# Order of products in a fused attention, MLP and expert kernel on one Trainium2 core: an up product moved across the group boundary, a transpose moved inside an expert tile, a weight split moved behind it

## The reference

```python
attn_out = _attn_ref(**attn_kwargs)          # 2 x 8 heads, 768 positions, head_dim 64; 8 global keys, 96 local ones
x = transpose(attn_out) -> (1536, 512)
h = x @ w_in                                 # (1536, 2048)
g = np.maximum(h, 0.0) + alpha * np.minimum(h, 0.0)
x = g @ w_out                                # (1536, 512)
logits = x @ w_gate + modality_bias[modality_id]     # 8 experts
e_idx = np.argmax(logits, axis=1)            # each token goes to one expert
gate_w = softmax(logits)[token, e_idx]
for e in range(8):
    mask = e_idx == e
    h = np.maximum(x[mask] @ w1[e], 0.0)     # 512 -> 1024
    out[mask] = gate_w[mask, None] * (h @ w2[e])     # 1024 -> 512
```

## Time and profile before

| what | value |
|---|---|
| median of 3 runs | 594.56 us (593.52 to 595.53) |
| the profiled execution's own time | 593.55 us |
| its span, first to last instruction | 591.8 us |
| PE busy | 577.8 us, 98% of the span |
| PE weight loads busy | 485.5 us, 82% |
| DVE busy | 331.5 us, 56% |
| ACT busy | 187.1 us, 32% |
| POOL busy | 122.0 us, 21% |
| mean granted TensorE clock | 0.997 |

### The profile page before, as it was taken

The page is one execution under the profiler, slowest core; times in us unless marked ns, Lnnn a source line. Parts: engine busy times, 40 slices in busy tenths (PEclk is TensorE's granted clock), DMA queues, the critical chain, the costliest instruction groups (busy, mean ns, idle before and its releaser), DMA issues.

```text
span 591.8 us, 10667 instructions
## 1 busy us (share of the span) xinstructions
PE 577.8 (98%) x3305; PEld 485.5 (82%) x3306; DVE 331.5 (56%) x852; ACT 187.1 (32%) x435; POOL 122.0 (21%) x187
## 2 busy tenths in 40 slices
PE   8999999999999999999999999999999999999995
PEld 4777778888989999899988999877778787877874
DVE  5877888787544465444554568775221289721211
ACT  4888887442010000100001004131221377521121
POOL 4444544997000000000000000101211113211110
PEclk9999999999999999999999999999999999999998
DMA  7976642562010000100001008014511169211110
GB/s 151 198 151 101 148 122 62 154 190 85 1 54 1 0 1 1 53 0 0 0 0 54 1 0 285 18 54 157 218 53 35 35 189 358 95 53 36 35 53 16
DMA packets 74544, 47.63 MB, mean 80 GB/s; under 512 B 52751, under 2 KB 60943, under 8 KB 74512
## 3 DMA queue, kind: packets, MB, share of 16 engines
q1 hardware_dynamic: 70288, 39.50, 23.9%
q0 software_dynamic: 2480, 7.34, 3.8%
q10 hardware_dynamic: 1744, 0.39, 0.3%
HBM read 40.93 MB, written 7.08 MB: 81 GB/s over the span
## 4 chain that ended last, share of the span: by engine, by line
PE 90%; DVE 5%; DMA 2%; issue 2%; ACT 1%; DVEq 0%
PE wide L1247 12%; PE wide L1249 11%; PE wide L1248 11%; PE wide L1235 9%; PE bank L1247 9%; PE bank L1249 9%; PE bank L1248 9%; PE bank L1407 4%; PE wide L1482 4%; PE bank L1507 4%; PE bank L1410 2%; DMA xg<-x_scratch,src_i 2%; PE wide L1346 2%; PE wide L1242 1%; PE bank L1495 1%
## 5 line engine op out<-in xcount | busy, mean ns | idle before, releaser
L865 DVE TENSOR_SCALAR h_act<-bank,alpha_sb 128x384 f32<-128x384 f32 x62 | 38.3, 617 | 106.3 <-PE bank L1249 106.3
L1247 PE MATMUL bank<-x_hl,wts 128*128 (+1 forms) x248 | 85.3, 344 | 0.0
L1249 PE MATMUL bank<-x_hl,wts 128*128 (+1 forms) x248 | 83.6, 337 | 0.0
L1248 PE MATMUL bank<-x_hl,wts 128*128 (+1 forms) x248 | 83.3, 336 | 0.0
L1247 PE MATMUL wide<-wts,h_h 128*128 128x512 f32 x192 | 75.7, 394 | 2.3 <-DVE h_l L868 2.3
L1249 PE MATMUL wide<-wts,h_l 128*128 128x512 f32 x192 | 75.9, 395 | 0.0
L1248 PE MATMUL wide<-wts,h_h 128*128 128x512 f32 x192 | 75.7, 394 | 0.0
L1124 DVE TENSOR_TENSOR hg_l<-wide,hg_h 128x256 fp32r<-128x256 f32 (+1 forms) x45 | 21.7, 510 | 59.8 <-ACT hg_h L605 59.5
L1247 PE MATMUL wide<-wts,hg_h 128*128 (+1 forms) x120 | 51.3, 427 | 0.2
L756 POOL DMA_INDIRECT xg<-x_scratch,source x1 | 1.9, 1920 | 226.9 <-DVE source L1021 226.9
L1247 PEld LDWEIGHTS bank<-x_hl,wts 128*128 128x128 f32 x248 | 46.6, 188 | 1.7
(11 more groups left out here) (217 smaller groups left out, 1040.0 us busy)
## 6 DMA issues: line engine op xcount, KB each, us to landing
stage<-in_moe_w SPq DMA_DIRECT2D x32, 512.0 KB, 7.5
ring<-in_moe_w_in SPq DMA_DIRECT2D x16, 256.0 KB, 2.9
ring<-in_moe_w_out SPq DMA_DIRECT2D x16, 256.0 KB, 2.9
v_raw<-in_v SPq DMA_DIRECT2D x16, 192.0 KB, 2.8
x_scratch<-x2row SPq DMA_DIRECT2D x4, 768.0 KB, 3.8
k_raw<-in_k SPq DMA_DIRECT2D x14, 192.0 KB, 3.3
q_raw<-in_q SPq DMA_DIRECT2D x14, 192.0 KB, 3.9
v_win<-in_v SPq DMA_DIRECT2D x16, 96.0 KB, 2.6
```

What stands on the lines that cost most here:

```text
L865: link(ts(h, acc, 0.0, alpha_sb[:, j:j + 1], ALU.min, ALU.mult))
L1247: pe.matmul(acc, lhs[0], rhs[0], start=start, stop=False)
L1248: pe.matmul(acc, lhs[0], rhs[1], start=False, stop=False)
L1249: return pe.matmul(acc, lhs[1], rhs[0], start=False, stop=stop)
```

## The change

```diff
@@ DVE, one expert tile
                 split(0)
                 hidden_low(t, 0)
-                split(1, 2)
+                split(1)
                 gathered_low(t + 1)
                 hidden_low(t, 1)
-                split(3, 4, 5, 6, 7)
+                split(2, 3, 4, 5, 6, 7)
                 scaled(t)
@@ PE, one MLP group
                     nxt = lambda j: up(g, j, order0[j] if first else j, banks[j % 2], first)
-                    if not first:
-                        nxt(0)
                     for j in range(FC):
                         if j + 1 < FC and not (first and j < 2 * AHEAD - 1):
                             nxt(j + 1)
+                        if j == FC - 1 and not last:
+                            up(g + 1, 0, 0, banks[0])
                         if j == 0:
                             pe.wait_ge(x2_copied, 2 * g + 2)
                         down(j)
@@ PE, one expert tile
                     pe.wait_ge(y_copied, t + 1)
                     pe.wait_ge(hg_low, 3 * t + 1)
-                    down_part(t, o, range(2))
+                    down_part(t, o, [0])
                     turn_h(t, 1)
-                    down_part(t, o, range(2, 4))
+                    down_part(t, o, range(1, 4))
                     pe.wait_ge(hg_low, 3 * t + 2)
```

## The result

| | before | after |
|---|---|---|
| median | 594.04 us (592.14 to 595.53, 4 runs) | 587.01 us (585.98 to 587.63, 4 runs) |
| profiled execution, its span | 593.55, 591.8 us | 586.40, 584.5 us |
| PE busy | 577.8 us | 570.6 us |

The ratio is 0.9886 with an interval of 0.9866 to 0.9905, that is 5.6 to 8.0 us. The direction is as forecast; the size is not: 7.0 us came off where 5.1 were forecast, and 587.01 lies 1.0 us under the low end of the range, 588.0. Of the 2.4 us between 587.01 and the 589.4 forecast, 0.5 come from the median of before, which a fourth run moved from 594.56 to 594.04.

The account below looks back on a forecast made before the run. The prediction took PE, busy 98% of the span, as the bound, so only gaps in its stream could pay. Gains of 2.8 + 2.1 + 0.2 = 5.1 us off 594.56 gave 589.4 us, range 588.0 to 592.0.

Parts of the forecast that it names:

- Part 2: Looped tiles: transposes three matmuls earlier close the stop at down chunk 4, 0.19 us in eleven ordinary tiles, 2.1 us.
- It is a wait: Down chunk 4 of looped tiles: the load, 0.30 us late, waits for DVE's low part, though the page says "issue".
- Part 1: MLP group boundaries: an up product moved across closes two stops, 0.94 us at each of three, 2.8 us.
- the copies' wait: Group boundary: ACT's accumulator copies, covered by up(1) alone, just fit; cost 0, bounds 0 and 0.3 us a boundary.
- The moved transposes: Looped tiles: ACT's hidden row reaches them in time; cost 0, bounds 0 and 0.1 us a tile.
- (b): Looped tiles: earlier transposes only move the wait and the tiles give nothing; 591.8 us, chance 0.10.
- (c): Group boundary: the wait for accumulator copies replaces both stops, and the tiles give nothing; 594.6 us, chance 0.08.
- Part 3: Three fresh tiles: split 2 later on DVE; together they give 0.2 us instead of 0.57.
- The refill: Fresh tiles: SP's later load of the next expert's piece 2 costs 0, upper bound 1.4 us.
- (a): Second fresh tile: the load of piece 2 is late by its upper bound, 1.4 us; 590.8 us, chance 0.10.
- (d): Second and third fresh tiles: a 12.6 us landing of SP's load stalls ACT 6.7 us each; 602.9 us, chance 0.04.

Follow-up runs that it names:

- e9_after_again: The kernel after, unchanged, run once more on the chip of the later runs: 588.05 us, ratio 0.9892.
- e6_after_load2: Kernel after with PE's table load at the head of each looped tile doubled: 590.51 us, ratio 0.9942.
- e7_before_flat: Kernel before with PE's tile loop written out with constant tile and expert numbers, no branch or table load: 590.72 us, ratio 0.9945.
- e10_after_pool: Kernel after with POOL issuing the next gather ahead of its wait for the scatter's landing: 585.34 us, ratio 0.9864.
- e11_after_scaled: Kernel after with DVE scaling the tile's output ahead of splits 6 and 7, POOL unchanged: 586.08 us, ratio 0.9868.
- e2_turn: Kernel before with only the transposes moved three matmuls earlier, DVE's splits unchanged: 589.32 us, ratio 0.9938.
- e3_tile: Kernel before with the earlier transposes and the later split 2, without the up product across the group boundary: 589.45 us, ratio 0.9937.
- e4_split: Kernel before with only DVE's split 2 moved behind the low part of the second half: 594.35 us, ratio 1.0015.
- e1_join: Kernel before with only the up product moved across the MLP group boundary: 590.09 us, ratio 0.9951.
- e12_after_pool_end: e10_after_pool with tile 0's first three up matmuls put ahead of the last group's last down product: 585.75 us, ratio 0.9866.
- e8_after_flat: Kernel after with PE's tile loop written out with constant tile and expert numbers: 586.86 us, ratio 0.9880.

## Why the prediction was too small

**The step that failed** is the sum of Part 2, "11 x 0.19 = 2.1 us": it counted one stop a tile where there were two. The waits of PE's weight loads had the second as plainly as the first, 3.5 us in 13 times against 4.6 in 13. I had read only a window around chunk 4, and so the price of the head of the next tile was missing. 0.35 us a tile were measured, 11 x 0.35 = 3.9 us, 1.8 more than forecast. The head's share, 0.16, is what is left of the 0.35 after the 0.19 of chunk 4. These 1.8 are nearly all of the 1.9 by which the gain of 7.0 is above 5.1; the other 0.5 of the distance from 589.4 is the median of before. The kernel after, run again as e9_after_again, gave 588.05 and a gain of 5.3 us, with an interval of 4.7 to 8.1 us that takes in the 5.1. So it is less the medians that show what was missing than the 12.30 us of the ordinary tiles, which all profiles with the turn but that of e6_after_load2 show.

**A reading in it was wrong as well.** The page said "issue" at chunk 4, and I wrote "It is a wait", since DVE's first low part ended some 0.2 ahead of the load. e7_before_flat shows that the page was nearer to the truth: most of the 0.30 was the sequencer's work behind the passed wait. The 0.19 for that stop came out right all the same, by luck: moving the transposes also passes the wait earlier, which gives the sequencer its time, whatever the lateness is made of.

**Part 1** held: 2.8 forecast, 2.96 in the profile, two stops gone at each of three boundaries, and the copies' wait at 0. The moved transposes cost 0 as forecast. So rivals (b) and (c) did not come true.

**Part 3** had its size about right, 0.2 against 0.02, but by luck: two large differences cancelled, and the reason was half wrong. That the gathered rows hold the third fresh tile is shown, by the chain and by two cures at two of its links (e10_after_pool, e11_after_scaled). That DVE holds PE in the second is not so. Before, DVE had a gap at that tile's start:

```profile
488.46 1.23 DVE L996 TENSOR_TENSOR wts<-stage,wts 128x1024 f32 x1 [0.36 <-issue]
```

In the kernel after it ran on there without one:

```profile
482.48 0.74 DVE L1129 TENSOR_SCALAR yrow<-wide,slot_gate 128x512 f32<-128x512 f32 x1
483.14 1.21 DVE L996 TENSOR_TENSOR wts<-stage,wts 128x1024 f32 x1
484.31 0.69 DVE L1124 TENSOR_TENSOR hg_l<-wide,hg_h 128x512 fp32r<-128x512 f32 x1
```

The first two fresh tiles took 12.3 us each and the third 13.4; 0.7 was won and lost again.

"Without this move Part 2's gain would be lost in these tiles" is half true. In e2_turn, without the move, the first two fresh tiles took 12.46 and 12.45 us, so of some 0.35 a tile they missed 0.15, and with the move they took 12.3. But the move also makes DVE's scaling later. In e2_turn it began 15.37 us behind the first fresh tile's first weight load (468.71), in the kernel after 16.04 us (466.44 to the 482.48 above):

```profile
484.08 0.75 DVE L1129 TENSOR_SCALAR yrow<-wide,slot_gate 128x512 f32<-128x512 f32 x1
```

The scatter and the gather hang on that scaling, and PE, with 0.3 us won in the first two tiles, is ready for the rows earlier: its wait for them was 0.6 us in e2_turn and 1.3 in the kernel after. So by the profiles the moved split took more than it gave while POOL's order stood: the three fresh tiles take 37.5 us without it and 38.0 with it, in both profiles of the kernel after. The medians of e2_turn and e3_tile do not separate the two. On the kernel before, alone, it lost as well (e4_split). Whether it pays with POOL's order of e10_after_pool was not run without the move, and stays open.

**The refill** was never late: ACT waits for no piece inside a fresh tile. Piece 2 was issued at 477.1 and landed in 3.9 us, and ACT took it at 482.38, 1.4 us later. It had 5.3 us to land; the prediction's 5.4 should have been 487.59 - 482.0 = 5.6 by its own rows, which changes nothing in the sum. Landings between 460 and 515 us took

```profile
DMA to landing us min/median/max: 3.9/6.1/7.3
```

Rivals (a) and (d) did not come true. The estimate of 3.2 us by the formula of the Trainium skill, "DMA: Bandwidth & Descriptors", section "Anatomy of one DMA", is still below the shortest of these. It stays open which landing would hurt, as no run had a late one.

**What is left open**: e1_join's and e2_turn's gains by medians (3.5 and 4.2) add up to 7.7, the change gave 7.0, each known to about 1 us; whether the two help or hinder each other by some tenths can't be told.

## What to carry to other kernels

In this kernel the gap marked "issue" at the head of the loop body is priced from the last wait of the body before: what the sequencer needs from there to the first instruction of the next round (here 1.7 us for step, branches and one table read, after the products still to be handed out) must be covered by work already handed out. Moving that last wait earlier, or writing the loop out, closes it, and a doubled table read shows within one run whether it binds. When a wait is closed in one place, count all groups of the engine's waits over the whole loop first, and look at transfers that are chained for no reason: a gather queued behind the landing of a scatter cost the kernel after 1.1 us by the profiles. e10_after_pool has the lowest median here, 585.34 us; e11_after_scaled and e12_after_pool_end lie within its interval.

## What the runs showed of the hardware

- One more reading of a number from a table by PE's sequencer cost 10.0 us in 14 tiles, 0.7 us each, where it was exposed; the table read itself is 0.3 us in the record (298 ns), so more than half of its price lies around it. With the kernel after's lead it cost 0.3 us a tile by the profiles.
- With matmuls 0.23 us apart, PE's sequencer stepped the loop at 533.0 while the matmuls up to 534.53 were still to run: it was 1.5 us ahead of them there, and needed 1.7. In the kernel after it was 2.0 us ahead (527.0, load due at 529.04), and the stop was gone.
- The same gather, from the same scratch, took 7.42 us beside the expert loads in the kernel after and 9.15 us in e3_tile. PE's wait behind it was 1.3 and 1.4 us in the two profiles of the kernel after, but 1.9 in e8_after_flat and 2.6 in e3_tile, whose order in the fresh tiles is the same. Such a wait should not be priced from one profile.
